# Attention keys of batch 0 loaded six rows to a partition, in a fused attention and mixture-of-experts kernel

## The reference

```
q, k, v: (2 batches, 8 heads, 768 tokens, 64)
k_sum = maximum of k over blocks of 32 tokens        # 24 summaries per head
v_sum = mean of v over blocks of 32 tokens
scores = q k^T / 8 inside a window (|i - j| < 16), and q k_sum^T / 8 + log(32)
a = softmax over both kinds of scores together;  x = a @ [v ; v_sum]
x -> (1536 tokens, 512);  h = x @ w_in (512 x 2048);  g = elu(h);  x = g @ w_out (2048 x 512)
router: cosine of x with 8 expert rows / tau, top 1 of 8, softmax gate
out = gate * (relu(x @ w1[e]) @ w2[e])               # w1 512 x 1024, w2 1024 x 512 for each expert
```

## Time and profile before

| | |
|---|---|
| median of three runs | 548.01 us |
| profiled execution | 549.35 us |
| span inside it | 547.7 us |
| TensorE busy | 534.2 us, 98% |
| VectorE busy | 303.0 us, 55% |
| ScalarE busy | 235.0 us, 43% |
| GpSimd busy | 83.7 us, 15% |

### The profile page before, as it was taken

One profiled execution on the slowest core, in us unless ns is written; L12 is line 12 of the kernel. 1 busy time (PEld: TensorE's weight loads), 2 busy tenths in 40 slices (PEclk: granted clock), 3 DMA queues, 4 the chain that ended last, 5 costly groups with the idle time before them and its releaser, 6 DMA issues.

```text
span 547.7 us, 11790 instructions
## 1 busy us (share of the span) xinstructions
PE 534.2 (98%) x3922; PEld 458.9 (84%) x3923; DVE 303.0 (55%) x672; ACT 235.0 (43%) x530; POOL 83.7 (15%) x210
## 2 busy tenths in 40 slices
PE   7899999999999999999999999999999999999995
PEld 7788888888888888888888898888788888888883
DVE  4678887544744465446543557667584274332552
ACT  5867764444544444444432345462171252211440
POOL 6313120011110000000000000110312222111221
PEclk9999999999999999999999999999999999999998
DMA  9999511222221112110100620010875155101000
GB/s 206 263 258 314 114 44 40 77 72 71 53 64 25 25 25 63 25 25 15 39 1 2 235 112 0 20 59 1 295 265 185 38 203 186 46 27 35 19 19 24
DMA packets 63499, 49.23 MB, mean 90 GB/s; under 512 B 46038, under 2 KB 52182, under 8 KB 63456
## 3 DMA queue, kind: packets, MB, share of 16 engines
q1 hardware_dynamic: 61056, 42.36, 26.7%
q0 software_dynamic: 2400, 6.30, 3.5%
HBM read 43.40 MB, written 6.82 MB: 92 GB/s over the span
## 4 chain that ended last, share of the span: by engine, by line
PE 91%; SPq 4%; DMA 2%; ACT 1%; issue 1%; DVE 0%; POOLq 0%; DVEq 0%; ACTq 0%
PE bank L937 24%; PE bank L979 8%; PE bank L986 8%; PE bank L992 8%; PE bank L1142 5%; PE bank L1188 5%; PE bank L1196 5%; PE bank L1150 5%; PE bank L1144 5%; PE bank L1190 5%; PE bank L1180 2%; PE bank L897 2%; PE bank L915 2%; PE bank L888 2%; DMA w_raw<-in_moe_w_out 2%; PE bank L1045 1%
## 5 line engine op out<-in xcount | busy, mean ns | idle before, releaser
L1346 ACT ACTIVATE el<-bank 128x512 f32<-128x512 f32 x48 | 28.6, 596 | 104.7 <-PE bank L937 104.5
L1633 DVE TENSOR_SCALAR el<-el 128x512 f32<-128x512 f32 x48 | 20.7, 430 | 87.3 <-ACT el L1346 87.3
L937 PE MATMUL bank<-x_hi,w_hi_parts 128*128 128x256 f32 x376 | 60.9, 283 | 0.0
L937 PE MATMUL bank<-x_hi,w_lo_parts 128*128 128x256 f32 x376 | 60.4, 282 | 0.0
L937 PE MATMUL bank<-x_lo,w_hi_parts 128*128 128x256 f32 x376 | 60.2, 282 | 0.0
L937 PEld LDWEIGHTS bank<-x_hi,w_hi_parts 128*128 128x128 f32 x376 | 53.6, 188 | 3.2 <-issue 0.2
L979 PE MATMUL bank<-w_hi_parts,g_hi 128*128 128x512 f32 x192 | 54.9, 407 | 0.6 <-ACT w_hi_parts L1340 0.6
L986 PE MATMUL bank<-w_lo_parts,g_hi 128*128 128x512 f32 x192 | 52.8, 397 | 0.0
L992 PE MATMUL bank<-w_hi_parts,g_lo 128*128 128x512 f32 x192 | 52.5, 395 | 0.0
L701 POOL COPY kb<-kT 128x96 f32<-128x96 f32 x96 | 26.8, 321 | 166.5 <-PE bank L888 142.9
L937 PEld LDWEIGHTS bank<-x_lo,w_hi_parts 128*128 128x128 f32 x376 | 51.5, 189 | 0.0
(11 more groups left out here) (271 smaller groups left out, 914.8 us busy)
## 6 DMA issues: line engine op xcount, KB each, us to landing
raw<-in_moe_w SPq DMA_DIRECT2D x8, 2048.0 KB, 9.3
w_raw<-in_moe_w_in SPq DMA_DIRECT2D x8, 512.0 KB, 7.6
w_raw<-in_moe_w_out SPq DMA_DIRECT2D x8, 512.0 KB, 8.0
k_raw<-in_k SPq DMA_DIRECT2D x16, 192.0 KB, 3.3
v_raw<-in_v SPq DMA_DIRECT2D x8, 384.0 KB, 4.3
x_rows<-x SPq DMA_DIRECT2D x6, 512.0 KB, 3.2
q_raw<-in_q SPq DMA_DIRECT2D x44, 64.0 KB, 2.9
vwin<-in_v SPq DMA_DIRECT2D x32, 72.0 KB, 2.3
```

Of the source, the lines that this page charges most:

```text
L937: mm = pe.matmul(o, r32(w[:, at:at + P]), r32(x[i % 2][:, c, :]), start=(part == "hh" and c == 0), stop=(part == "lh" and c == DC - 1))
L1346: act.activation(el[n % 2], bank[:, H_BANK[n % 2], :], ACT.Exp).then_inc(e_act, 1)
```

## The change

Keys of batch 0 are loaded like the values: partition p gets tokens 6p to 6p + 5, 1536 bytes in one run for each head, both heads in one load (4 loads in place of 8). Turning such a tile needs 128x64 pieces (one head, one of the six tokens of each partition), and the two heads' outputs go to the two halves of the partitions, so each of the three transposes of a half becomes two ordinary products with the unit matrix (24 products to a pair are not transposes any more: 12 products, two passes each). The columns come out sorted by token within the partition, so ScalarE's copy writes them six elements apart. Besides: `fill` is 6 and 3 products instead of 11 and 4; w_in(0) is issued ahead of windows 2 and 3; ScalarE stores x of unit 1 and splits w_in(0) ahead of the copies of `means(3)` and unit 3's probabilities, and VectorE splits w_in(0) behind x of unit 1; for n = -1 and 0 the splits of weights come behind `g_high(n + 1)`; and `route_turn(3, 1)` moves from place 71 to 73.

```diff
     def r_at(i, t):
-        return PER_BLOCK * (i + 1) + 3 + 4 * t
+        return PER_BLOCK * (i + 1) + (9 if (i, t) == (NB - 3, 1) else 3 + 4 * t)
             def load_k0(g):
-                load_keys(2 * g, k_raw0[:, g, :], ld_k0[g])
+                sp.dma_start(k_raw0[:, g, :].rearrange("p (h n) -> p h n", h=2),
+                             kh[2 * g:2 * g + 2].rearrange("h (p t) d -> p h (t d)", p=P)).then_inc(ld_k0[g], 16)
             load_windows(1)
+            load_w_in(0)
             load_windows(2)
             load_windows(3)
-            load_w_in(0)
-                    pe.wait_ge(ld_k0[g], 32)
+                    pe.wait_ge(ld_k0[g], 16)
                 for t in range(KT // 2):
-                    at = (a * (KT // 2) + t) * P
-                    mm = pe.transpose(o[:, t * P:(t + 1) * P], src[:, at:at + P], ident[:, :])
+                    at = a * (KT // 2) + t
+                    if batch == 1:
+                        mm = pe.transpose(o[:, t * P:(t + 1) * P], src[:, at * P:(at + 1) * P], ident[:, :])
+                    else:
+                        for h in range(2):
+                            mm = pe.matmul(o[h * D:(h + 1) * D, t * P:(t + 1) * P],
+                                           src.rearrange("p (h t d) -> p h t d", h=2, d=D)[:, h, at, :], ident[:, :],
+                                           start=True, stop=True)
-            fill(11)
+            fill(6)
             keys_and_queries(0)
-            fill(4)
+            fill(3)
-                act.copy(kT[:, g, at:at + S // 2], bank[:, b, 0:S // 2]).then_inc(k_ev, 1)
+                if batch == 0:
+                    some = slice(a * (KT // 2), (a + 1) * (KT // 2))
+                    act.copy(kT[:, g, HALO:HALO + S].rearrange("p (n t) -> p t n", t=KT)[:, some, :],
+                             bank[:, b, 0:S // 2].rearrange("p (t n) -> p t n", n=P)).then_inc(k_ev, 1)
+                else:
+                    act.copy(kT[:, g, at:at + S // 2], bank[:, b, 0:S // 2]).then_inc(k_ev, 1)
             evacuate_p(2)
+            store_x_high(1)
+            split_high("in", 0)
             evacuate_first_means(3)
             evacuate_p(3)
-            store_x_high(1)
-            split_high("in", 0)
                 elu_exp(n + 1)
-                for part in HIGH_STEPS.get(n, ()):
-                    split_high(*part)
+                if n > 0:
+                    for part in HIGH_STEPS.get(n, ()):
+                        split_high(*part)
                 behind(2 * n - 1)
                 g_high(n + 1)
+                if n <= 0:
+                    for part in HIGH_STEPS[n]:
+                        split_high(*part)
             store_x_low(1)
+            split_low("in", 0)
             store_x_low(2)
             store_x_low(3)
-            split_low("in", 0)
```

## The result

The changed kernel takes 547.79 us (median of 20 runs) where the kernel before takes 548.76: a ratio of 0.9977 with a 95% interval of 0.9966 to 0.9987. By the ratio it is 1.26 us or 0.23% faster, by the two medians 0.97 us. The forecast was 545.4 us, 2.6 us less. The profiled execution took 547.92 us (549.35 before), its span 546.2 (547.7 before); these two executions differ by 1.43 us.

The account below looks back on a forecast made before the run. TensorE, busy 534.2 of 547.7 us, bounds the kernel; VectorE leads the front. Terms -0.35 - 0.65 - 0.93 - 0.48 - 0.2 = -2.6 us from the 548.01 median give 545.4 us, own range 544.7 to 546.2 (chance 0.52).

Parts of the forecast that it names:

- Part 3, "Front: -0.35": Fills and front: shorter fills end as keys land, maxima of pair 1 start at 8.5: -0.35 us (-1.2 to +0.6).
- Part 4: ScalarE's copies of keys to elements 24 bytes apart: no extra time taken, +0.3 us a copy kept for a rival.
- Start of pair 1: In the front: pair 1's keys land by 6.2 us and are turned from 6.5 to 7.9 us.
- the rival of the strided copies: ScalarE's eight key copies each cost +0.3 us, VectorE gains nothing: -1.65 us, 546.4 us; chance 0.14.
- Turning: TensorE's turning of keys: 24 overlapping passes at 0.055 us, 1.3 us a pair, 0.65 more (bounds 0.65 to 1.95).
- Part 5: End of the front: store and split of w_in(0) fill ScalarE's gap, values(3) starts at 24.95 us: -0.65 us.
- Part 6: g_high ahead of the splits for n = -1 and 0, idle in 32 to 36 and at 41 us goes: -0.93 and -0.48.
- The landing of the queries by 31.9: Condition at project(0): queries of unit 5 land near 31.9 us with SyncE 2.0 us earlier, 0.6 us of margin.
- place 73: Moving the router's turn removes TensorE's wait at L897 for the router's copy: -0.2 us.
- only the reorderings work: Rival: longer turning leads the front by 0.6 us, queries of unit 5 come no earlier: -1.25 us, 546.8; chance 0.14.
- The halves don't overlap: Slower rival: turning keys takes 24 passes at 0.11 us, L897 is 3.9 us later: +1.6 us, 549.6; chance 0.08.
- The transfer that would hide the gain of the windows: Windows 2 and 3, issued behind 512 KB more, come late and values(2) takes back the end-of-front gain; expected in time.

Follow-up runs that it names:

- number 1: Changed kernel with the 11 and 4 fill products of before instead of 6 and 3: 548.78 us, ratio 0.9991 to the kernel before.
- number 4: Kernel before with the key path alone (loads, products, strided copies, fills 6 and 3), all reorderings and place 73 undone: 548.72 us, ratio 1.0002.
- number 5: Changed kernel with ScalarE's splits of n = -1 and 0 ahead of g_high again: 547.92 us, ratio 0.9988 to the kernel before.
- Number 6: Changed kernel with two key loads a pair again, one a head, in the long rows: 548.45 us, ratio 0.9998 to the kernel before.
- number 2: Changed kernel with ScalarE's copies of batch 0 keys written side by side, so it computes something else: 547.37 us, ratio 0.9967 to the kernel before.
- number 7: Kernel before with the reorderings alone, plus the queries of unit 5 issued ahead of w_in(2): 547.47 us, ratio 0.9982 to the kernel before.
- number 3: Kernel before with the reorderings alone, place 73 included; keys, products and fills as before: 547.74 us, ratio 0.9973 to the kernel before.
- number 9: Kernel before with the reorderings, queries of unit 5 issued earlier, and keys of pair g + 1 issued ahead of queries of pair g: 547.86 us, ratio 0.9989.
- number 8: The changed kernel run once more, unchanged: 547.32 us, ratio 0.997 to the kernel before.
- number 12: Changed kernel with TensorE sorting columns, copies side by side, next pair's keys issued ahead of queries, no fills after pair 0: 546.75 us, ratio 0.996.
- numbers 10 and 11: Changed kernel with TensorE sorting the columns and ScalarE copying side by side, run twice: 546.91 us, ratio 0.9968, then 547.56 us, ratio 0.9985.

## Why the prediction was wrong

The sign was right, the size was not: half or less of what was forecast came. **The step that failed is Part 3, "Front: -0.35"**, and with it Part 4, taken at nothing. The front came 1.72 us later. The reading that VectorE leads from the maxima of pair 1 on held: the first L897 came 5.63 us after their start in the kernel before and the first L905 5.75 after it in the changed one (10.52 to 16.27). In six traces with the changed key path (the changed kernel twice, numbers 1, 4, 5 and 6) it comes 8.22 to 8.23 us after the start of pair 1, whenever that is. What failed is the start of these maxima: 8.5 forecast, 10.52 measured. Against the forecast 14.2 for L905 the 2.07 us split so:

- *Start of pair 1*: 6.5 forecast, 8.04 measured (+1.54). Pair 1's keys landed 4.7 us after their issue at 2.39, at 7.1, not at 6.2; number 4, in which the clock was no trouble, starts there (7.07): 0.57 of it. The other 0.97 is the clock. The prediction took the moment of its rise, 4.5 us, from one trace. With the same 12 fill passes ahead, the 24 passes of pair 0 took 2.83 and 2.52 us in the changed kernel's two traces, and 2.69, 2.32, 2.24 and 1.54 in numbers 6, 2, 5 and 4. The slowest group ran at (2.83 less the 0.42 of one) / 23 = 0.105 us a pass (1.2 GHz), the others reach (1.53 - 0.27) / 23 = 0.055 (2.4); by these paces the rise lies between 4.3 and 7.0 us. A late rise does not need the shorter fills: 22 passes in a row took 4.30 and 4.31 (number 7), but also 4.75 (number 3), 4.78 (number 1) and 5.06 us (number 9). Whether the shorter fills or the new products delay it on average, these traces can't tell. The clock column prints 1.00 all through. With 11 fills the keys started after the rise in four of five traces; with 6 they take what is left of the slow clock upon themselves, and the two-pass products lose up to 1.3 us by it, where the six transposes of number 9 lost 0.5.
- *Copies*: the strided write costs 0.39 us each, more than the rival's bound of 0.3, and 0.43 on the path (number 2). So the rival of the strided copies was real and came on top of the rest. The Trainium skill (SBUF — State Buffer, the note on cachelines) says that each access that crosses to a new 16-byte line pays a penalty, and the trace agrees: 0.87 us against 0.48.
- *Turning*: 7.80 us from pair 1 to the first L905 in number 2, 7.11 in the kernel before: +0.69 where +0.59 was taken. The pace of 0.055 us a pass was exact.

Two of the prediction's own signs of being wrong stand in the trace: copies above 0.6 us, and slow weight loads after 5 us (230 ns each up to 6.4 us, 137 from 8 us on).

Part 5 (-0.65) was right: -0.67, and -0.66 in number 3.

Part 6 forecast 1.41 us and 2.05 came (1.41 before `project(0)` and 0.64 behind it), mostly by another cause. It gave the 0.38 us before `project(0)` to the earlier queries, but the 0.55 of `g_high(0)` and the 0.48 at 41 us to the order of the splits. Number 3, with the order and without the earlier transfers, gains nothing there, since the queries of unit 5 land late; number 4, with the transfers and without the order, gains 1.38 of the 1.41 before `project(0)` (3.12 us from `hidden(1)` against 4.50) and 0.48 behind it; number 5 puts the order at 0.17 us. Both waits before `project(0)` were waits for transfers: w_out(1) was issued at 22.50 and landed 8.2 us later, at 30.7, where in the kernel before it landed at 33.2.

```profile
w_raw<-in_moe_w_out SPq DMA_DIRECT2D x1, 512.0 KB, 8.2
```

Number 6 shows that the four issues saved on SyncE are needed for it. The landing of the queries by 31.9 stood in the prediction as a condition with 0.6 us of margin; early transfers were the cause. The terms came out larger than the idle read from the earlier trace rows, 1.41 against 0.93, 0.64 against 0.48 and 0.35 against 0.2 for place 73: the reading is that a stop also takes the overlap of the last product's end with the next product, 0.15 to 0.25 us each time, and two stops lay before `project(0)`. No run tests this reading.

Of the rivals, "only the reorderings work" named the number (-1.25), and by the measured times its name holds too: the reorderings alone (ratio 0.9973) give as much as the whole change (0.9977, and 0.997 in number 8), the key path alone gives nothing (1.0002). Its mechanism is not what happened. It priced the front at +0.6, where +1.72 came, and kept 0.4 us of wait for the queries of unit 5, which went. That the number fits is luck. "The halves don't overlap" is excluded by the pace. The transfer that would hide the gain of the windows (Part 5) didn't occur.

In the traces the key path loses 0.73 us at the front (`hidden(1)` at 31.14 in number 4, 30.41 before) and gives back 1.38 between `hidden(1)` and `project(0)`; the reorderings win 0.66 at the front and, alone, lose 0.55 of it again in a longer wait at `project(0)`.

One more part of the distance lies in the yardstick. The forecast started from 548.01, the median of three runs; over 20 runs the kernel before takes 548.76, so that 0.75 of the 2.4 us between 545.4 and 547.79 were there before any change. The profiled execution of before, 549.35, lies 0.6 above its median over 20 runs and shows the waits of 32 to 42 us at a size that many executions may not have; what an average execution waits there was not measured.

## What to carry to other kernels

When a load is rearranged to save issues, follow the layout through to the last reader: here the strided copy and the two-pass products ate what the loads gave. Letting TensorE write the sorted order gave back 0.26 of the copy's 0.43 us (number 12), which the times don't yet set apart from the changed kernel. Where a chain of loads feeds waits 20 us later, ask of each reordering whether the next operand would have landed by then; and where work is moved into the first 7 us, price it at the slow clock as well, since its rise moves from execution to execution. And try the parts of a change one by one: here the key path, the larger part of the work, added nothing that the measurement shows.

## What the runs showed of the hardware

- TensorE's rise from 1.2 to 2.4 GHz came between about 4.3 and 7.0 us of the span, in programs that had run products without a stop of more than 0.3 us since 1.3 us, and at different times in the same program (2.83 and 2.52 us for the same 24 passes in the changed kernel, 2.12 and 2.83 for the same 48 in numbers 10 and 11).
- ScalarE's copy of 384 float32 columns from a bank takes 0.48 us to adjacent elements and 0.87 us to elements 24 bytes apart. TensorE's writes to a bank 24 bytes apart go at full pace (0.029 us a pass of 64 columns, two halves of the columns in turn; 0.031 side by side).
- A stop of 0.39 and 1.26 us came after the same pass of 48 short ones in two traces of one kernel. The profile names no releaser. It ended 1.7 us after the end of an "instruction" transfer both times; that this is the cause is not shown.
